# Gating logits of the first five chunks with the gate weights standing in four column quarters

## The reference

```python
# 1 attention with decay: B=4, H=8, S=576, head 64
scores = (1 / sqrt(64)) * q @ k.T ;  ret = (scores * Dmat) @ v        # Dmat: gamma**(i-j), lower triangle
x = ret.transpose(0, 2, 1, 3).reshape(2304, 512)
# 2 dense feed-forward, 512 -> 2048 -> 512
h = x @ w_in ;  g = max(h, 0) + log1p(exp(-abs(h))) ;  x = g @ w_out
# 3 mixture of 8 experts, the best 2 of each token
logits = x @ w_gate
noisy  = logits + log1p(exp(x @ w_noise)) * noise                     # [2304, 8] each
top2   = two largest of noisy per token; weights = softmax over the two
out[token] += weight * (max(x[token] @ w1[e], 0) @ w2[e])             # 512 -> 1024 -> 512
```

## Time and profile before

| | |
|---|---|
| median of 3 runs | 1028.63 us (1027.62 to 1030.16) |
| the profiled execution | 1028.34 us, of it 1026.5 us between its first and last instruction |
| TensorE busy | 1007.9 us, 98% of the span |
| VectorE, ScalarE, GpSimd busy | 39%, 42%, 20% |
| mean granted TensorE clock | 0.996 of full |

### The profile page before, as it was taken

The page is one execution under the profiler, slowest core; times in us unless marked ns, Lnnn a source line. Parts: engine busy times, 40 slices in busy tenths (PEclk is TensorE's granted clock), DMA queues, the critical chain, the costliest instruction groups (busy, mean ns, idle before and its releaser), DMA issues.

```text
span 1026.5 us, 22021 instructions
## 1 busy us (share of the span) xinstructions
PE 1007.9 (98%) x5982; PEld 874.2 (85%) x5983; DVE 396.6 (39%) x784; ACT 430.6 (42%) x736; POOL 208.4 (20%) x198
## 2 busy tenths in 40 slices
PE   9999999999999999999999999999998999999996
PEld 7889999999999999999887888888887888888885
DVE  3565632432532423436553222242366354222221
ACT  3337754544545445557532222242354354222221
POOL 4540000020110200200332222222323222322222
PEclk9999999999999999999999999999999999999999
DMA  8754450000000000053216211244277342211111
GB/s 276 246 167 126 150 186 1 1 32 0 0 31 0 0 31 0 31 185 123 83 25 216 80 61 57 72 131 138 87 244 252 120 130 95 78 59 52 52 47 45
DMA packets 47076, 95.24 MB, mean 93 GB/s; under 512 B 19245, under 2 KB 24749, under 8 KB 42928
## 3 DMA queue, kind: packets, MB, share of 16 engines
q1 hardware_dynamic: 24240, 66.26, 18.9%
q0 software_dynamic: 10992, 27.84, 8.6%
q10 hardware_dynamic: 11808, 0.68, 0.7%
HBM read 78.98 MB, written 20.37 MB: 97 GB/s over the span
## 4 chain that ended last, share of the span: by engine, by line
PE 94%; DMA 2%; issue 2%; ACTq 1%; POOL 0%; ACT 0%; DVE 0%; DVEq 0%; SPq 0%; POOLq 0%
PE bank L697 27%; PE bank L699 27%; PE bank L698 27%; PE bank L829 3%; PE bank L776 2%; PE bank L648 2%; PE bank L622 2%; PE bank L752 1%; PE bank L641 1%; DMA xg<-x_rows,meta_x 1%; PE bank L608 1%; PE bank L661 1%; PE bank L746 1%; DMA out<-ysb,meta_y 1%; DMA kdec<-c_k 0%
## 5 line engine op out<-in xcount | busy, mean ns | idle before, releaser
L697 PE MATMUL bank<-ew,hT_hi 128*128 (+1 forms) x328 | 132.1, 403 | 2.4 <-DVE hT_lo L1415 2.3
L697 PE MATMUL bank<-ew,xgT_hi 128*128 (+1 forms) x328 | 132.0, 402 | 0.0
L697 PE MATMUL bank<-xs_hi,mw 128*128 (+1 forms) x384 | 130.0, 338 | 0.0
L699 PE MATMUL bank<-xs_hi,mw 128*128 (+1 forms) x384 | 129.6, 337 | 0.0
L698 PE MATMUL bank<-xs_lo,mw 128*128 (+1 forms) x384 | 129.0, 336 | 0.0
L699 PE MATMUL bank<-ew,hT_lo 128*128 (+1 forms) x328 | 128.7, 392 | 0.0
L699 PE MATMUL bank<-ew,xgT_lo 128*128 (+1 forms) x328 | 128.7, 392 | 0.0
L698 PE MATMUL bank<-ew,xgT_hi 128*128 (+1 forms) x328 | 128.6, 392 | 0.0
L698 PE MATMUL bank<-ew,hT_hi 128*128 (+1 forms) x328 | 128.5, 392 | 0.0
L516 POOL DMA_INDIRECT lists<-rec,slot x36 | 35.7, 991 | 391.4 <-DVE slot L1319 382.3
L697 PE MATMUL bank<-mw,g_hi 128*128 128x512 f32 x288 | 115.0, 399 | 0.0
(11 more groups left out here) (179 smaller groups left out, 1688.7 us busy)
## 6 DMA issues: line engine op xcount, KB each, us to landing
raw<-w_ex SPq DMA_DIRECT2D x32, 1024.0 KB, 4.8
stage<-w_ff SPq DMA_DIRECT2D x16, 512.0 KB, 3.3
out<-blank SPq DMA_DIRECT2D x3, 1536.0 KB, 11.0
x_rows<-x2sb SPq DMA_DIRECT2D x6, 768.0 KB, 3.6
kbuf<-kN SPq DMA_DIRECT2D x16, 256.0 KB, 2.9
vbuf<-vN SPq DMA_DIRECT2D x16, 256.0 KB, 4.5
qbuf<-qT SPq DMA_DIRECT2D x15, 256.0 KB, 3.9
xg<-x_rows,meta_x POOLq DMA_INDIRECT x43, 3.6
```

The source lines that it names most:

```text
L697: pe.matmul(o, a_hi, b_hi, start=first, stop=False)
L699: return pe.matmul(o, a_lo, b_hi, start=False, stop=last)
```

## The change

- TensorE transposes the three tiles in three consecutive steps, 2, 3 and 4. The transposed rows of the whole chunk are kept: `x2T` is now three tiles wide and lies in the part of `xs_hi` that is out of use (for the last of the five in `xs_lo`'s place).
- A transpose of tile j now waits for the copy of tile j-1 (`x2T_kept`), where it waited for the copy of the logits.
- Step 5, `gate_products`: four float32 matmuls, one for each 128 features. The weights standing are 32 columns (the 16 of the gate and 16 of zeros), placed in the k-th quarter of the array's columns; the 384 token rows move. The result goes to partitions 32k to 32k+31 of `gate_ps`.
- ScalarE copies the 384 columns to `lgT`.
- Step 6, `gate_logits`: for each tile one float32 matmul with 128 columns of `lgT` standing and a 0/1 matrix of 16 columns moving (`small[:, 8:24]`), which sums the four quarters and turns the result back to tokens on partitions.
- VectorE copies all three tiles' logits at once, in step 8.
- ScalarE's piece of the gate moves into `soft`, between Ln and the wait for `g_done`. It has the three copies in steps 4, 5, 6 and the copy of the products in step 7.
- TensorE's loop over chunks 1 to 4 becomes two rounds of two written-out chunks.

```diff
+    small[:, 8:24] = i[:, None] % 32 == np.arange(16)
...
             def gate_transpose(c, j):
...
-                pe.wait_ge(gate_kept, c * TJ + j)
+                else:
+                    pe.wait_ge(x2T_kept, c * TJ + j)
                 for k in range(KT):
                     last = pe.transpose(gate_ps[:, k * P:(k + 1) * P], x2sb[:, j, k * P:(k + 1) * P], ident)
                 last.then_inc(x2T_made, 1)

-            def gate_logits(c, j):
-                pe.wait_ge(x2T_kept, c * TJ + j + 1)
+            def gate_products(c, par):
+
+                pe.wait_ge(x2T_kept, c * TJ + TJ)
                 for k in range(KT):
-                    last = pe.matmul(gate_ps[:, 0:16], x2T[:, k, :], wg[:, k, :], start=(k == 0), stop=(k == KT - 1))
-                last.then_inc(gate_made, 1)
+                    last = pe.matmul(gate_ps[32 * k:32 * k + 32, 0:TOK], wg[:, k, :], (x2T_late if par is None else x2T_in[:, par])[:, k, :],
+                                     start=True, stop=True, tile_position=(0, 32 * k), skip_group_check=True)
+                last.then_inc(lgT_made, 1)
+
+            def gate_logits(c):
+
+                pe.wait_ge(lgT_kept, c + 1)
+                for j in range(TJ):
+                    last = pe.matmul(gate_ps[:, 16 * j:16 * j + 16], lgT[:, j * P:(j + 1) * P], small[:, 8:24],
+                                     start=True, stop=True)
+                last.then_inc(gate_made, TJ)
...
-            def gate_part(c, f):
-                if f in (2, 4, 6):
-                    gate_transpose(c, (f - 2) // 2)
-                elif f in (3, 5, 7):
-                    gate_logits(c, (f - 3) // 2)
+            def gate_part(c, f, par):
+                if f in (2, 3, 4):
+                    gate_transpose(c, f - 2)
+                elif f == 5:
+                    gate_products(c, par)
+                elif f == 6:
+                    gate_logits(c)
...
-            with pe.Fori(1, NCH - 1) as c:
-                ff_chunk(c, True, True)
-            ff_chunk(NCH - 1, True, False)
+            with pe.Fori(0, (NCH - 2) // 2) as i:
+                for u in range(2):
+                    ff_chunk(2 * i + u + 1, True, True, u)
+            ff_chunk(NCH - 1, True, False, None)
...
                 nc.scalar.activation(t, t, ACT.Ln, bias=1.0).then_inc(log_done, 1)
+                if gate:
+                    gate_part(c - 1, f)
                 act.wait_ge(g_done, n + 1)
...
             def keep_x2T(c, j):
                 act.wait_ge(x2T_made, c * TJ + j + 1)
-                act.wait_ge(gate_made, c * TJ + j)
-                nc.scalar.activation(x2T[:, :, :], gate_ps[:, :].rearrange("p (k n) -> p k n", k=KT), ACT.Copy
+                nc.scalar.activation(x2T(c)[:, :, j * P:(j + 1) * P],
+                                     gate_ps[:, :].rearrange("p (k n) -> p k n", k=KT), ACT.Copy
                                      ).then_inc(x2T_kept, 1)
+
+            def keep_products(c):
+                act.wait_ge(lgT_made, c + 1)
+                nc.scalar.activation(lgT[:, 0:TOK], gate_ps[:, 0:TOK], ACT.Copy).then_inc(lgT_kept, 1)
...
-                if f in (3, 5, 7):
-                    keep_x2T(c, (f - 3) // 2)
+                if f in (4, 5, 6):
+                    keep_x2T(c, f - 4)
+                elif f == 7:
+                    keep_products(c)
                 elif f == 8:
                     gate_noise(c)
...
-            def keep_logits(c, j):
-                dve.wait_ge(gate_made, c * TJ + j + 1)
+            def keep_logits(c):
+                dve.wait_ge(gate_made, c * TJ + TJ)
                 at_least(dve, gate_step, c * GATE_STEPS)
-                dve.tensor_copy(lg[:, j, :], gate_ps[:, 0:16]).then_inc(gate_kept, 1)
+                dve.tensor_copy(lg[:, :, :], gate_ps[:, 0:16 * TJ].rearrange("p (j n) -> p j n", j=TJ)
+                                ).then_inc(gate_kept, TJ)
...
-                if f in (4, 6, 8):
-                    keep_logits(c, (f - 4) // 2)
+                if f == 8:
+                    keep_logits(c)
```

More of the change, by code:

```diff
@@ L141, in build @@
         xs_hi, a = place("xs_hi", [P, 2, KT, TOK], F32R, R_T)
+        x2T_in, _ = place("x2T_in", [P, 2, KT, TOK], F32, R_T)
+        x2T_late, _ = place("x2T_late", [P, KT, TOK], F32, R_T + 2 * KT * TOK * 4)
         xs_lo, a = place("xs_lo", [P, 2, KT, TOK], F32R, a)
@@ L148, in build @@
         x2sb, a = place("x2sb", [P, TJ, D], F32, R_S)
-        x2T, R_C = place("x2T", [P, KT, P], F32, a)
+        lgT, R_C = place("lgT", [P, 512], F32, a)
         decay, a = place("decay", [P, 2, PAIRS, P], F32, R_T + 3 * KT * TOK * 4)
@@ L169, in build @@
         ident, earlier, allrows = square[:, 0, :], square[:, 1, :], square[:, 2, :]
-        wg, a = place("wg", [P, KT, 16], F32, a)
+        wg, a = place("wg", [P, KT, 32], F32, a)
         noi, a = place("noi", [P, TILES, E], F32, a)
@@ L281, in build @@
         x2T_made, x2T_kept, gate_made, gate_kept = (sem(n) for n in ("x2T_made", "x2T_kept", "gate_made", "gate_kept"))
+        lgT_made, lgT_kept = sem("lgT_made"), sem("lgT_kept")
         gate_exp, gate_log = sem("gate_exp"), sem("gate_log")
@@ L314, in as32, with x2T @@
             return ap.bitcast(F32)
+        def x2T(c):
+            if isinstance(c, int):
+                return x2T_late
+            return x2T_in[:, bass.ds(c % 2, 1), :, :].rearrange("p o k n -> p (o k) n")
         def q_of(t):
@@ L777, in tile_transpose, with ff_chunk @@
                 last.then_inc(xgT_made, 1)
-            def ff_chunk(c, gate, more):
+            def ff_chunk(c, gate, more, par=0):
                 for f in range(FT1):
@@ L787, in ff_chunk @@
                     if gate:
-                        gate_part(c - 1, f)
+                        gate_part(c - 1, f, par)
                     ff_out(c, f)
@@ L866, in last_gate_logits @@
                     for k in range(KT):
-                        last = pe.matmul(gate_ps[:, 16 * j:16 * j + 16], x2T_end[:, j, k, :], wg[:, k, :],
+                        last = pe.matmul(gate_ps[:, 16 * j:16 * j + 16], x2T_end[:, j, k, :], wg[:, k, 0:16],
                                          start=(k == 0), stop=(k == KT - 1))
@@ L971, in split_x, with soft @@
                                      xT[:, :, bass.ds(c * TOK, TOK)], ACT.Copy).then_inc(xs_hi_done, 1)
-            def soft(c, f):
+            def soft(c, f, gate):
                 n, t = c * FT1 + f, act_t[:, f % 2, :]
@@ L1019, in ff_chunk @@
                         split_piece(f + 2, f % 2)
-                    if gate:
-                        gate_part(c - 1, f)
-                    soft(c, f)
+                    soft(c, f, gate)
                     if f == 0 and not (isinstance(c, int) and c == 0):
@@ L1590 @@
             moe_w_out.reshape(FT1, P, D)], axis=2)),
-        "w_gn": pack(np.concatenate([moe2_w_gate, moe2_w_noise], axis=1)),
+        "w_gn": pack(np.concatenate([moe2_w_gate, moe2_w_noise, np.zeros((D, 16), np.float32)], axis=1)),
         "noise": pack(moe2_noise.reshape(TILES, P, E).transpose(1, 0, 2)),
```

## The result

The kernel after takes 1031.15 us (median of 12 runs, 1030.19 to 1033.58), beside 1028.72 for the kernel before on the same chip (12 runs, 1025.97 to 1030.53). The ratio is 1.0025, 95% interval 1.0015 to 1.0036. The forecast was 1030.3, within 0.3% of no change, and so it came out. But of the 2.4 us, only 0.8 are where the forecast had 1.7.

The account below looks back on a forecast made before the run. TensorE, busy 1007.9 of 1026.5 us, was taken as the bound. Per chunk 0.78 + 1.25 + 1.00 - 2.70 = +0.33 us, +1.7 for five, gave 1030.0, or 1030.3 for the median; own range 1028 to 1032.5, overall 1026.6 to 1034.4.

Parts of the forecast that it names:

- The bound and the stage: Gated chunks, 155 to 512 us: TensorE's instructions stand end to end, so every 0.1 us in its order counts.
- The four waits: Per chunk TensorE waits for ScalarE's copies: transposes of tiles 1 and 2 (0.33 late each), products, summing product (0.22 late).
- The copy at T + 1.77: T is TensorE's start of a step; ScalarE's copy starts behind Ln at T + 1.77, lasts 0.60, ends at T + 2.37.
- The products: Step 5: eight records in four column quarters at once take 0.65 us; with waiting, entering and leaving, 1.25 per chunk.
- rivals 2 and 3: Products: two column groups at a time, +0.65 per chunk, 1033.6, chance 0.14; quarters one after another, +1.95, 1040.1, chance 0.05.
- Leaving the form of use: TensorE's change back from the column-quarter products to ordinary matmuls: 0.20 us, within 0.09 to 0.20.
- Entering: TensorE's change into the column-quarter form before the products: 0.09 us, swallowed by the wait, plus a first gap 0.05 longer.
- The summing product: Step 6: 0.22 us late, 0.11 for an unhidden weight load, 0.67 for six records; 1.00 us per chunk.
- The sum: Per chunk 0.78 + 1.25 + 1.00 - 2.70 = +0.33 us; +1.7 for five chunks.
- Rival 1: ScalarE's copies are ready by T + 2.07, so no waits; five chunks save 5.1 us, 1023.5; chance 0.10.
- After the gate all hangs on TensorE as before and moves along: Stages behind the gate: they only shift in time with TensorE; no cost of their own in the sum.
- The clock stretch: Half-clock stretches near 510 and 796 us may move or drop; 1.7 us allowed on both sides.

Follow-up runs that it names:

- copies_early: Kernel after, with ScalarE's copies of steps 4 to 7 ahead of the step's Abs instead of behind its Ln; ratio to the kernel before 0.9955.
- before_page: Kernel before, with TensorE's loop written as two rounds of two chunks and 216 unused semaphore increments in the first chunk; ratio to before 1.0032.
- before_unrolled: Kernel before, with only TensorE's loop over chunks 1 to 4 written as two rounds of two chunks; ratio to before 1.0000.
- two_quarters: Kernel after, with the four products in two column quarters, two summed in each; ratio to the kernel before 1.0062.
- rolled: Kernel after, with TensorE's loop back to one chunk per round and x2T at a fixed place; ratio to the kernel before 1.0015.
- one_quarter: Kernel after, with all four products in one column quarter, summed there one after another; ratio to the kernel before 1.0117.

## Why the prediction was right, and where it was not

**The bound and the stage.** Right. TensorE is without a gap in the gate stage but for the 20 waits, and each tenth in its order is a tenth of the chunk.

**The four waits.** Right in place, number and cause; copies_early takes them away and nothing else takes their place. The copy at T + 1.77 came out as chained. Two sizes were off. The copy took 0.58, not 0.60, and from its end to TensorE's next start 0.05 us passed (304.72 to 304.77), where I took 0.07: the wait is 0.29 instead of 0.33 (0.47 between the starts, where 0.175 is usual). So the transposes cost 0.35 each, not 0.39. This is the term that was mis-sized most, because it counts four times.

**The products.** Four quarters at once: right, and rivals 2 and 3 are out; the kernels that enforce them cost +0.74 and +2.05 per chunk, where the prediction had +0.65 and +1.95. The block costs 1.18 us instead of 1.25: 0.04 less for the wait and 0.03 less inside, where the first gap is 0.02 longer and not 0.05. Leaving the form of use was right at 0.20, from the attention rows. From the last start to the next main matmul there are 0.42 us, of which the record itself is 0.32, and the gap behind that is 0.34 instead of 0.23. Entering was right too: in copies_early, where no wait hides it, the products start 0.27 us after the last `ff_in` record, 0.09 more than is usual.

**The summing product.** 0.96 instead of 1.00: 0.19 of waiting instead of 0.22, the rest as worked out.

**The sum.** 0.35 x 2 + 1.18 + 0.96 = 2.84 us per chunk, against the old three pieces. These, by the same reading of starts, were 2.68, not 2.70. That makes +0.16, as the distances give it. The forecast of +0.33 is too high by four small errors on the same side, nearly all of it the length of the four waits. For five chunks it is 0.8 us instead of 1.7.

**Rival 1** (the copies are in time) was wrong for this kernel, but its price was right within some tenths: 5.1 us were to be saved, and the chunks of copies_early save 5 x 1.05 = 5.3. By the ratio of 0.9955 the whole kernel saves 4.6. That its median of 1023.61 us all but equals the forecast's 1023.5 is chance, since before took 1027.12 beside it and not 1028.63.

**What carries the median to 1031.15.** "After the gate all hangs on TensorE as before and moves along" was the step that failed. In the traces the expert stage adds the longer wait near 540 us; a shift of when instructions come in was nowhere in the sum. The clock stretch was allowed for, on both sides. In the trace of before one lies at 509.4 us and one at 796.1; in that of after at 542.3 and 798.3. Such a stretch costs 1.6 us. From tile 2 to tile 3 there are 13.94 us with the one at 542.3 and 12.34 without. From the ranks of the fifth chunk to those of the sixth there are 26.2 to 26.3 us in the five traces with a stretch between them (it begins at 503 to 515 us) and 24.6 to 24.7 in the other eight, and the wait near 540 us does not take that up: the last record is issued 9.2 us behind the ranks with the stretch and without it, so what TensorE waits for comes as much later. This trace's 3.1 us is 0.8 from the gate, 1.9 from the longer wait, 1.6 from the stretch at 542.3, less the 1.6 of the stretch that before has at 509.4, and some tenths that weren't traced. The prediction puts both stretches of before down to idle time of TensorE, but its rows show that for the one near 796 only; ahead of the one at 509.4 TensorE had been busy since 499.4. That the forecast lay only 0.9 us under the median is partly luck: a gate term 0.9 too high stood in for a cost that it didn't know.

## What to carry to other kernels

When a result is copied by one engine and used by another in the same step, chain the starts on the copying engine to the tenth of a microsecond: here 0.3 us, four times per chunk, was more than the whole gain, and moving the copy ahead of that engine's own wait, where nothing kept it, gave it back. A narrow standing operand pays on TensorE by filling the other columns with work of the same kind, which cost one turn, not four. After any change of an engine's instruction count, look at stages that the diff doesn't touch, and compare the distances there over more than one trace before explaining them.

## What the runs showed of the hardware

- **Four column quarters with all 128 rows, each with a stream of its own, run at full concurrency:** eight records with 384 moving columns take 0.85 us in four quarters, 1.48 in two, 2.77 in one. Entering the form costs 0.09 us where no wait hides it (copies_early, 0.27 instead of 0.175 between two starts), and leaving it 0.09 (0.42 where a record takes 0.32). The page "TensorEngine Tiling (Array Packing)" of the Trainium skill, section Key Properties, says that changing the tiling mode drains TensorE; the traces agree in that both changes cost time, and don't show that it is a drain.
- **Instructions come in pages over the same DMA engines as small transfers.** A page for TensorE near 530 us (16 KB, one packet on one DMA engine) took 1.2 and 1.35 us in the two traces of before and 2.5 to 3.4 in the others; why, stays open. In the five traces where it overlapped such a store long, 30 packets of a 32-packet store went out within 0.2 us, and the last two only when the page ended (in after 529.73 us, the page's end 529.74). SyncE's load behind the store then came 4.5 to 5.2 us after its first packets, and 3.4 to 3.9 otherwise.
- **Instructions put in ahead of a loop can change how the loop itself is fetched.** The loop of before_page is that of before_unrolled; only the first chunk, ahead of it, has 216 increments more. Yet pages come through the whole loop, where before_unrolled has none from 282 to 448 us, and in one chunk TensorE stands for 1.84 and 2.96 us, with four pages in 16 us. That it stood for lack of instructions is argued; why only in that chunk stays open.
- **Stretches of half clock** (granted clock at 1.2 instead of 2.4 GHz, 3.4 us long, costing 1.6) follow the wait near 540 us in after (twice), copies_early, two_quarters and rolled, but not in the other eight traces. The four first are those in which TensorE stood longest there, 3.6 to 3.9 us in two parts. But the wait's length alone doesn't decide it: rolled stood for 2.1 us and has a stretch, one_quarter for 2.6 and has none. What does, stays open.
